# A fused attention and two gated layers on one core: the first weights' split moved to other units, and x and one copy of turned probabilities ahead of exponentials

## The reference

```python
def _attn_ref(q, k, v, n_global, n_local):          # 8 global keys, 96 local ones
    scores = scale * np.matmul(q, k.transpose(0, 1, 3, 2))
    ...
    scores = scores + bias[None, :, :, :]           # -slope of the head * distance
    scores = np.where(keep, scores, -1000000000.0)
    scores = scores - np.max(scores, axis=-1, keepdims=True)
    a = np.exp(scores)
    a = a / (np.sum(a, axis=-1, keepdims=True) + 1e-09)
    return np.matmul(a, v).astype(np.float32)

def _moe_ref(x, w_in, conv_w, w_out):
    h = np.maximum(x @ w_in, 0.0)
    ...                                             # conv_out: three taps of h along the sequence
    gate = 1.0 / (1.0 + np.exp(-conv_out))
    return (h * gate @ w_out).astype(np.float32)

def _moe2_ref(x, w_in, w_spatial, b_spatial, w_out):
    h = np.maximum(x @ w_in, 0.0)
    u, v = (h[..., :d_ff // 2], h[..., d_ff // 2:])
    ...                                             # v_n: v normalised over its features
    v_s = np.einsum('ts,bsd->btd', w_spatial, v_n) + b_spatial[None, :, None]
    return ((u * v_s) @ w_out).astype(np.float32)
```

## Time and profile before

| | before |
|---|---|
| median of 3 runs | 360.92 us (360.45 to 361.19) |
| profiled execution | 360.66 us, span 358.9 us |
| granted TensorE clock, mean | 0.999 |
| PE, DVE, ACT, POOL busy | 352.8, 216.3, 177.8, 90.0 us |
| the chain of work that ended last, by engine | PE 87%, DVE 5%, POOL 4%, ACT 3% |

### The profile page before, as it was taken

The page is one execution under the profiler, slowest core; times in us unless marked ns, Lnnn a source line. Parts: engine busy times, 40 slices in busy tenths (PEclk is TensorE's granted clock), DMA queues, the critical chain, the costliest instruction groups (busy, mean ns, idle before and its releaser), DMA issues.

```text
span 358.9 us, 7396 instructions
## 1 busy us (share of the span) xinstructions
PE 352.8 (98%) x2890; PEld 322.4 (90%) x2891; DVE 216.3 (60%) x572; ACT 177.8 (50%) x451; POOL 90.0 (25%) x165
## 2 busy tenths in 40 slices
PE   8999999999999999999999999999999999999996
PEld 4658998998899999999889999998999999998885
DVE  6996898778785797889693942115853444441000
ACT  4987677776676688562464622114652111112112
POOL 4889897445553000000120300003400000000000
PEclk9999999999999999999999999999999999999999
DMA  7962442333314033312000000010340000001222
GB/s 207 398 248 73 121 132 68 128 101 113 112 46 162 2 117 120 117 30 89 0 2 1 2 0 0 2 44 1 119 150 28 0 0 2 0 2 60 106 100 95
DMA packets 12233, 27.77 MB, mean 77 GB/s; under 512 B 1568, under 2 KB 4256, under 8 KB 12192
## 3 DMA queue, kind: packets, MB, share of 16 engines
q1 hardware_dynamic: 11904, 27.10, 22.5%
q10 hardware_dynamic: 288, 0.13, 0.2%
HBM read 24.08 MB, written 3.15 MB: 76 GB/s over the span
## 4 chain that ended last, share of the span: by engine, by line
PE 87%; DVE 5%; POOL 4%; ACT 3%; issue 1%; DVEq 0%; ACTq 0%; POOLq 0%
PE bank L1588 20%; PE bank L1590 20%; PE bank L1589 20%; PE bank L1544 15%; PE bank L1523 4%; PE bank L1499 3%; PE bank L1453 2%; POOL p_sb L635 2%; ACT p_sb L735 2%; DVE p_sb L1073 2%; POOL w_lo L652 1%; PE bank L1555 1%; DVE denom L1082 1%; DVE c_sb L1110 1%; POOL w_hi L647 1%
## 5 line engine op out<-in xcount | busy, mean ns | idle before, releaser
L1544 PE MATMUL bank<-xT,w_hi 128*128 128x384 f32 x256 | 69.6, 345 | 0.1
L635 POOL TENSOR_SCALAR p_sb<-p_sb,denom 128x256 f32<-128x256 f32 (+1 forms) x96 | 47.9, 511 | 35.7 <-DVE denom L1084 35.7
L735 ACT ACTIVATE p_sb<-p_sb,row_min 128x256 f32<-128x256 f32 (+1 forms) x96 | 46.5, 490 | 14.9 <-DVE row_min L1073 14.9
L1544 PEld LDWEIGHTS bank<-xT,w_hi 128*128 128x128 f32 x256 | 45.7, 188 | 0.8 <-issue 0.5
L1544 PE MATMUL bank<-xT,w_lo 128*128 128x384 f32 x128 | 44.1, 344 | 0.0
L1110 DVE SCALAR_TENSOR_TENSOR c_sb<-h_sb,conv_sb,c_sb 128x382 f32<-128x382 f32 (+1 forms) x64 | 42.1, 658 | 2.3
L1588 PE MATMUL bank<-g_hi,w_hi 128*128 128x386 f32 (+1 forms) x128 | 43.3, 338 | 0.0
L1590 PE MATMUL bank<-g_hi,w_lo 128*128 128x386 f32 (+1 forms) x128 | 43.2, 337 | 0.0
L1589 PE MATMUL bank<-g_lo,w_hi 128*128 128x386 f32 (+1 forms) x128 | 43.1, 336 | 0.0
L656 POOL TENSOR_SCALAR rstd<-mean_var 128x1 f32<-128x1 f32 x12 | 4.7, 390 | 129.2 <-DVE mean_var L1138 129.2
L1073 DVE CUSTOM_DVE_ANT_0 p_sb<-bank,table 128x256 f32<-128x256 f32 (+1 forms) x96 | 33.0, 398 | 4.6 <-PE bank L1453 4.6
(11 more groups left out here) (96 smaller groups left out, 786.3 us busy)
## 6 DMA issues: line engine op xcount, KB each, us to landing
stage<-in_weights SPq DMA_DIRECT2D x17, 512.0 KB, 3.3
v_sb<-in_v SPq DMA_DIRECT2D x8, 390.0 KB, 3.8
k_sb<-in_k SPq DMA_DIRECT2D x8, 384.0 KB, 4.1
out_dram<-out_sb SPq DMA_DIRECT2D x11, 256.0 KB, 2.0
q_sb<-in_q SPq DMA_DIRECT2D x13, 192.0 KB, 2.4
v_sb<-in_v SPq DMA_DIRECT2D x6, 260.0 KB, 4.0
k_sb<-in_k SPq DMA_DIRECT2D x5, 256.0 KB, 2.9
stage_late<-in_weights SPq DMA_DIRECT2D x2, 512.0 KB, 11.2
```

Source lines behind the costliest of these rows:

```text
L635: nc.gpsimd.tensor_scalar(probs_h, probs_h, denom[:, u % SLOTS, h:h + 1], 1.0, ALU.mult, ALU.mult).then_inc(scaled, 1)
L735: nc.scalar.activation(p_sb[:, u % SLOTS, h, 0:n], p_sb[:, u % SLOTS, h, 0:n], ACT.Exp, bias=row_min[:, u % SLOTS, h:h + 1], scale=-1.0, a ...
L1544: last = nc.tensor.matmul(h_bank(j)[:, 0:C], w, x, start=r == 0, stop=r == F1_GROUP - 1)
```

## The change

It has two parts. On GpSimd, piece 3 of the first weights (counted from 0) is split behind unit 15, where it was behind 16; pieces 4 and 5 are split behind unit 17, where they were behind 17 and 19; pieces 6 and 7 behind unit 20, where they were behind 20 and 22. In triple 4, ScalarE rounds x of triple 3 and copies unit 12's turned probabilities ahead of the exponentials of units 15 and 16, where they stood behind those of unit 15, the copy first. VectorE takes the remainder of that x behind the bias of unit 15, where it stood behind those of 15, 16 and 17.

```diff
-ROUND_AFTER = {6: 1, 13: 1, 14: 1, 16: 1, 17: 1, 19: 1, 20: 1, 22: 1}
-REST_AFTER = {8: 1, 13: 1, 14: 1, 16: 1, 17: 1, 19: 1, 20: 1, 22: 1}
+ROUND_AFTER = {6: 1, 13: 1, 14: 1, 15: 1, 17: 2, 20: 2}
+REST_AFTER = {8: 1, 13: 1, 14: 1, 15: 1, 17: 2, 20: 2}
...
             for p in range(HP, ALL_TRIPLES):
                 u = TG * p
+
+                if p == F1_FIRST:
+                    round_x(p - 1)
+                    copy_pt(u)
                 for tt in range(TG):
                     if p + 1 < ALL_TRIPLES:
                         soften(u + TG + tt)
                     if tt == 2:
                         relu_h(2 * (p - F1_FIRST))
-                    copy_pt(u + tt)
-                    if tt == 0:
+                    if p > F1_FIRST or tt > 0:
+                        copy_pt(u + tt)
+                    if tt == 0 and p > F1_FIRST:
                         round_x(p - 1)
...
                     if p + 1 < ALL_TRIPLES:
                         bias_scores(u + TG + tt)
-                rest_of_x(p - 1)
+                    if tt == 0 and p == F1_FIRST:
+                        rest_of_x(p - 1)
+                if p > F1_FIRST:
+                    rest_of_x(p - 1)
```

## The result

Over 22 runs of each the changed kernel takes 361.32 us (360.66 to 362.0), the kernel before 360.84 us (360.41 to 361.32). The ratio is 1.0016 with a 95% interval of 1.0010 to 1.0022: slower by 0.48 us between the medians (0.58 by the ratio), where I had forecast 0.1 less. The time lies in my range, but the change went the other way.

What follows compares the result with a forecast made beforehand. TensorE was taken as the bound, its useful idle time lying before unit 24. Old stalls -0.87, new ones +0.15, +0.3, +0.3 and +0.05 gave -0.07, some -0.1: 360.92 to 360.8 us, range 360.1 to 361.6.

Steps and rivals of the forecast that it cites:

- What bounds the kernel: TensorE, busy 352.8 of 358.9 us: only its idle time can be saved, and what counts lies before unit 24.
- x and the copy: Triple 4: the 0.33 us stall goes, unit 14 newly waits 0.15 for unit 13's copy; TensorE leaves 0.18 earlier.
- Piece 3 behind 15: Triple 5: unit 16 is scaled at 37.32, 0.4 us before TensorE turns it, so the move is free.
- The first pair: Pieces 4 and 5 together behind unit 17: unit 21's biases start at 43.95, 0.65 us later; new stall 0.3.
- the wait for unit 18's scaling: Triple 6: scaling ends about 44.25, after TensorE wants its second half; new stall 0.3 us.
- just fits: Triple 6: unit 18's copy ends at 46.0, unit 19's transposes want it at 46.1, so no stall.
- The second pair: Pieces 6 and 7 together behind unit 20: new stalls of 0.3 us for unit 21's scaling and 0.05 for its copy.
- The gains in triples 6 and 7: The old stalls there, 0.54 us together, go, as piece 7 is ready early and unit 23 is scaled by about 55.1.
- the port is held whole: Slow rival, chance 0.13: multiply-adds can't run beside the rounds either, 0.6 us more per pair; 1.75 new stalls, 361.8 us.

Runs made afterwards that it cites:

- the second profile of the kernel before: The kernel before, unchanged, run and profiled again; ratio 0.9998, its four triples summing to 33.59 us.
- the tables alone: The kernel before with only the new split places of pieces 3 to 7, x and the copy unmoved; ratio 1.0018, 0.65 us slower.
- rounds ahead on the kernel before: The kernel before with rounds from piece 5 on one piece ahead of their remainders, remainders apart, x and copy unmoved; ratio 0.9987.
- the last variants: Rounds ahead, remainders apart: changed kernel 0.9985, with piece 3 behind unit 15 0.9989, kernel before 0.9987; changed kernel with more rounds ahead and unit 13's copy moved 0.9977.

## Why the prediction was wrong

*What bounds the kernel.* Right. TensorE's idle time ahead of unit 24 was all that moved.

*x and the copy.* Right in mechanism and place: rounding at 28.04, unit 13 without a wait, a new wait of unit 14 for ScalarE. The net gain was 0.23 against 0.18 forecast, and the new wait 0.10 against 0.15; against the second profile of the kernel before the gain would be 0.78, so that the 0.23 comes close is in part luck. The exponentials that came 0.2 later cost nothing. (The two instructions pass the two exponentials of unit 15, not four; the times of the prediction fit two.)

*Piece 3 behind 15.* Free, as forecast: triple 5 is 8.10 in every kernel that I read.

*The first pair.* This is the step that failed, in the words of the prediction: "the next tap's simple operation slips in at the change, the second remainder holds the multiply-add until 42.85". What slips in at the change from one remainder to the next is the operation on the sums, which had been standing since 40.48. The simple operation comes behind it and its reciprocal, so it is the one that stands for the second remainder (1.29 us), and both multiply-adds still lie ahead when it is over. I had laid the operation on the sums and the simple one in one gap. The biases of unit 21 came at 44.59 instead of 43.95. Half of these 0.64 us is this extra multiply-add: from the end of the hold to the biases it took 1.42 us (43.17 to 44.59), where I had 1.10. The other half is that the hold ended at 43.17 and not at 42.85, in an execution in which TensorE too was 0.26 later than I had it (unit 18 at 44.16 and not 43.90), and in which the two rounds took 1.60 us beside the taps, where I had 1.2.

Counted from TensorE's start on unit 18, the biases came 0.43 behind it, where I had 0.05. And the wait for unit 18's scaling, which I had priced at 0.3 and which would have held TensorE back, didn't come: the scaling ended at 44.26, as forecast, only 0.1 after TensorE's start, and the first half covered it. So TensorE was at unit 19 without that delay, and the copy of unit 18, which "just fits" by 0.1, came too late by 0.60 (0.38 + 0.3 - 0.1, within 0.02). Triple 6 cost 0.66 where I had 0.3, and by another wait.

*The second pair.* Forecast 0.35 in all (0.3 for the scaling of unit 21, 0.05 for the copy of unit 21). Triple 7 is 0.49 above its undisturbed length. By the starts it is 2.33 - 1.90 = 0.43 in front of unit 22's transposes, 0.12 of it at the transposes of unit 21 (0.78 instead of 0.66; the second half of that unit was scaled only at 51.87 + 1.29 = 53.16), the rest, 0.31, in the wait for the copy. The waits are the two that I named, but the shares are the wrong way round, and the copy began at 54.59 where I had 53.6 to 54.0.

*The gains in triples 6 and 7.* Both old stalls went, as forecast. The four triples don't hold quite the same matmuls, as I had written; by the undisturbed length of 8.05 the stalls were worth 0.64 and not 0.54.

In sum: 0.97 of old stalls went, and 0.10 + 0.66 + 0.49 = 1.25 came, where I had 0.87 and 0.80. That the time still lies in the range says little for the working, since the range held gains and losses alike. What a measurement tells from no change I had put at 0.2%; this one resolved 0.06%, and shows the change of 0.16% as a loss.

The slow rival, "the port is held whole", had the direction right. The taps' first multiply-adds did lose time beside the two rounds, 1.72 us for the pair instead of 1.27, a loss of 0.45 where the rival had 0.6; but its sum of 1.75 us of new stalls is above the 1.25 that came. By the Trainium skill ("SBUF — State Buffer", section "SBUF: two separate sides") the pair of ports that GpSimd and VectorE share is locked for the whole instruction, and the other engine fully blocks. Beside remainders the trace agrees (1.26, 1.29 and 3.07 us). I had called scalings milder than that; the count above shows them to be shorter, not milder.

What stays open: against the first profile of the kernel before, the triples give the change 0.28 us and the measurement 0.48, with an interval from 0.36 to 0.79. On the same footing the kernels that have the x move (ten profiles) came out 0 to 0.5 us slower in the measured time than their triples say, 0.2 in the mean; the two variants without it (the tables alone, rounds ahead on the kernel before) agree within 0.1. The scatter of the start of unit 12 is larger than this, and one or two profiles of each kernel can't settle where it goes. So how much the x move is worth in the measured time is not shown. Also open is whether GpSimd's operations hold VectorE by their length alone, as the rows suggest, or by their two inputs as well: remainders split into short pieces with both inputs kept would tell, and were not run.

## What to carry to other kernels

A long operation of GpSimd (here a remainder: two inputs, 1.29 us) was a closed door for VectorE's simple operations and multiply-adds, whatever their own length. What counted was not the length of VectorE's work but the number of times that it came to the door: the chain of short dependent operations (sums, reciprocal, next tap) lost a whole remainder twice over, and multiply-adds of 8 columns did no better than that. So put such operations of GpSimd apart, and under stretches in which VectorE reads from the banks (the six biases of the changed kernel between 34.60 and 36.75 took 0.42 us each, the last three of them beside a remainder that ran from 35.47), and let the shorter rounds run ahead in the gaps, as the last variants did. When a forecast ends with a margin of 0.1 us that "just fits", the step ahead of it has to be laid out instruction by instruction, since a slip there is the result. And before a difference between two profiles is explained, profile the unchanged kernel twice.

## What the runs showed of the hardware

Beside 2.83 us of remainders the small operation on the sums and the simple operation took 1.26 and 1.29 us, beside 2.98 us of short operations with one input 0.30 and 0.38. Beside two remainders a pair of multiply-adds took 3.07 us with 382 columns and 2.38 with 8, where the same pairs take 1.27 and 0.49 with GpSimd idle. Where two remainders stood in a row, the change between them let in the one operation of VectorE that was waiting (it ended at 41.74); the simple operation behind its reciprocal, recorded from 41.88 on, stood 1.29 us. And the start-up of one and the same program scatters by the time the first layer begins: unit 12 came at 26.82 and 27.55 us in two profiled executions of the kernel before, and at 26.8 to 28.3 over all profiles. In triple 4 the kernel before lost 0.55 us of the earlier start again.
